# Attention projection by copied token halves, and folds moved to GpSimd

## The reference, cut to what matters

```
def _attn_ref(q, k, v, w_phi):                 # q, k, v: (4, 8, 576, 64), w_phi: (64, 128)
    def phi(x):
        proj = np.einsum('bhsd,df->bhsf', x, w_phi)
        proj = proj - np.max(np.abs(proj), axis=-1, keepdims=True)
        return np.concatenate([np.exp(proj), np.exp(-proj)], axis=-1)
    q_p, k_p = (phi(q), phi(k))
    kv = np.einsum('bhsf,bhsd->bhfd', k_p, v)
    z = np.sum(k_p, axis=2)
    num = np.einsum('bhsf,bhfd->bhsd', q_p, kv)
    den = np.einsum('bhsf,bhf->bhs', q_p, z)[..., None] + 1e-06
    return (num / den).astype(np.float32)
def reference(**kwargs):                       # sequence 576, model width 512
    attention, then x = x + real(fft2(x)) and a channel MLP of width 2048 over its normed rows,
    then a token MLP of width 256, then a channel MLP of width 1536
```

## Time and profile before

| | us |
|---|---|
| median of 3 runs | 994.19 (993.21 to 994.72) |
| the profiled execution's own time | 993.24 |
| its span in the trace | 991.4 |
| PE busy | 976.3 (98%) |
| PE weight loads busy | 879.4 (89%) |
| DVE, ACT, POOL busy | 380.3, 285.3, 181.6 |

### The profile page before, as it was taken

One profiled execution on the slowest core, in us unless ns is written; L12 is line 12 of the kernel. 1 busy time (PEld: TensorE's weight loads), 2 busy tenths in 40 slices (PEclk: granted clock), 3 DMA queues, 4 the chain that ended last, 5 costly groups with the idle time before them and its releaser, 6 DMA issues.

```text
span 991.4 us, 17316 instructions
## 1 busy us (share of the span) xinstructions
PE 976.3 (98%) x7275; PEld 879.4 (89%) x7275; DVE 380.3 (38%) x758; ACT 285.3 (29%) x573; POOL 181.6 (18%) x159
## 2 busy tenths in 40 slices
PE   8999999999999999999999999999999999999998
PEld 6999999888899999899899999788999999999997
DVE  6998888851421322313213213463121212121211
ACT  6865756633311111111111112353111111111110
POOL 3653555369500000000000000136000000000000
PEclk9999999999999999999999999999999999999999
DMA  7232241435310010010100300695010101000000
GB/s 230 80 111 55 74 130 48 165 110 166 108 64 1 1 64 1 1 63 0 37 26 0 105 7 1 208 322 197 1 64 1 64 1 51 13 33 30 32 1 32
DMA packets 48398, 66.88 MB, mean 67 GB/s; under 512 B 22864, under 2 KB 23888, under 8 KB 48208
## 3 DMA queue, kind: packets, MB, share of 16 engines
q1 hardware_dynamic: 46608, 59.69, 18.6%
q10 hardware_dynamic: 1728, 6.29, 1.7%
HBM read 47.10 MB, written 18.87 MB: 67 GB/s over the span
## 4 chain that ended last, share of the span: by engine, by line
PE 73%; POOL 2%; DMA 1%; DVE 1%; ACT 0%; issue 0%; SPq 0%; POOLq 0%
PE mlp_y L1086 11%; PE mlp_y L1087 11%; PE mlp_hid L1073 11%; PE mlp_hid L1071 11%; PE mlp_hid L1072 11%; PE mlp_y L1085 11%; PE mlp_turn_in L1056 1%; PE tok_y L1387 1%; PE tok_y L1389 1%; PE tok_y L1388 1%; POOL mlp_w_lo L1033 1%; DMA mlp_w_raw<-in_w_mlp 1%; PE tok_hid L1389 1%; PE tok_hid L1388 1%; PE tok_hid L1387 1%; DMA tok_w<-in_w_tok 0%
## 5 line engine op out<-in xcount | busy, mean ns | idle before, releaser
L1204 DVE SCALAR_TENSOR_TENSOR mlp_h_lo<-mlp_hid,mlp_h_hi 128x384 fp32r<-128x384 f32 x168 | 93.7, 558 | 465.1 <-ACT mlp_h_hi L1121 465.0
L1071 PE MATMUL mlp_hid<-mlp_ut_hi,mlp_w_hi 128*128 128x384 f32 x672 | 229.1, 341 | 0.5 <-POOL mlp_w_lo L1033 0.5
L1121 ACT ACTIVATE mlp_h_hi<-mlp_hid 128x384 fp32r<-128x384 f32 x168 | 82.7, 492 | 502.9 <-PE mlp_hid L1073 502.9
L1073 PE MATMUL mlp_hid<-mlp_ut_hi,mlp_w_lo 128*128 128x384 f32 x672 | 226.5, 337 | 0.0
L1072 PE MATMUL mlp_hid<-mlp_ut_lo,mlp_w_hi 128*128 128x384 f32 x672 | 225.4, 335 | 0.0
L1085 PE MATMUL mlp_y<-mlp_w_hi,mlp_h_hi 128*128 128x512 f32 x504 | 197.3, 391 | 3.0 <-DVE mlp_h_lo L1204 2.9
L1087 PE MATMUL mlp_y<-mlp_w_hi,mlp_h_lo 128*128 128x512 f32 x504 | 199.4, 396 | 0.0
L1086 PE MATMUL mlp_y<-mlp_w_lo,mlp_h_hi 128*128 128x512 f32 x504 | 198.9, 395 | 0.0
L1033 POOL TENSOR_TENSOR mlp_w_lo<-mlp_w_raw,mlp_w_hi 128x1024 fp32r<-128x1024 f32 x26 | 61.7, 2395 | 402.9 <-ACT mlp_w_hi L1282 381.6
L1071 PEld LDWEIGHTS mlp_hid<-mlp_ut_hi,mlp_w_hi 128*128 128x128 f32 x672 | 126.3, 188 | 6.6 <-issue 1.2
L1072 PEld LDWEIGHTS mlp_hid<-mlp_ut_lo,mlp_w_hi 128*128 128x128 f32 x672 | 126.3, 188 | 5.2
(11 more groups left out here) (146 smaller groups left out, 1081.9 us busy)
## 6 DMA issues: line engine op xcount, KB each, us to landing
mlp_u<-u_scratch SPq DMA_DIRECT2D x12, 768.0 KB, 4.6
mlp_w_raw<-in_w_mlp SPq DMA_DIRECT2D x14, 512.0 KB, 5.2
mlp_w_raw<-in_w_mlp ACTq DMA_DIRECT2D x12, 512.0 KB, 6.0
v<-in_v SPq DMA_DIRECT2D x16, 320.0 KB, 3.6
qk<-in_kT SPq DMA_DIRECT2D x16, 288.0 KB, 4.1
qk<-in_qT SPq DMA_DIRECT2D x15, 288.0 KB, 4.2
u_scratch<-x_all SPq DMA_DIRECT2D x4, 1024.0 KB, 4.9
x_scratch<-mlp_u SPq DMA_DIRECT2D x5, 768.0 KB, 3.6
```

The source lines that it names most:

```text
L1071: nc.tensor.matmul(out, w_hi[:, j, col], hi, start=(c == 0), stop=False)
L1073: last = nc.tensor.matmul(out, w_lo[:, nf - 1 - j, col], hi, start=False, stop=(c == DC - 1))
L1121: nc.scalar.activation(h_hi[:, j % 2, :], hid[j % 2][:, 0:BT], ACT.Relu).then_inc(h_rounded, 1)
L1204: nc.vector.scalar_tensor_tensor(out=h_lo[:, j % 2, :], in0=hid[j % 2][:, 0:BT], scalar=0.0, in1=h_hi[:, j % 2, :], op0=ALU.max, op1=ALU.s ...
```

## The change

The projection of every pair but the first takes another form. SP copies the rounded tokens of each head, from the 64 rows where they lie, to both halves of the 128 rows of new buffers (`rest_twice`, `key_twice`, `query_twice`): four transfers for each of three groups, twelve for a pair. A new weight matrix `wphi_both` has the high part over the low part, 128 rows by 128 columns. A tile is now multiplied in three products: low tokens by `wphi_hi` (256 columns, as before), and for each head its copied tokens by `wphi_both` (128 columns each). PE waits for the copies of REST, of the keys and of the queries. `rest_twice` has two buffers, the others one.

DVE's two folds of `x_all` go to POOL (`pool_fold`), but for the last pair's. POOL's additions of one batch's results move: the second from steps k % 4 = 0 to 1, the third and the row from 1 to 2, the latter two ahead of the fold. SP stores the first batch at pair 13 in place of 11, and the second behind the load of the first MLP's block.

PE's queue in step 0, from the first projection of pair 1 on: before, each tile has three products of 256 columns (L299 is the third).

Two folds came in, and the addition went to the next step. The diff, without the lines that only follow from it:

```
--- before.py
+++ after.py
@@ -116,6 +116,13 @@
+    wphi_both = at("wphi_both", [128, F], F32R, 157824)
+    rest_twice = at("rest_twice", [128, 2, 2, 128], F32R, 134912)
+    key_twice = at("key_twice", [128, 2, 512], F32R, 130816)
+    query_twice = at("query_twice", [128, 2, 512], F32R, 77824)
...
@@ -151,6 +158,9 @@
+    rest_copied = [sem("rest_copied0"), sem("rest_copied1")]
+    key_copied = sem("key_copied")
+    query_copied = sem("query_copied")
...
@@ -236,6 +242,25 @@
         else:
             sp.wait_ge(ones_set, 3)
         sp.dma_start(v[:, p.parity, :, :, 0:DH], dram["v"][p.n]).then_inc(v_loaded[p.parity], 16)
+    def copy_twice(sp, p, first, to, done):
+        for h in range(2):
+            for half in range(2):
+                from_ = qk_hi[DH * h:DH * h + DH, p.parity, first:first + to.shape[2]]
+                sp.dma_start(to[64 * half:64 * half + 64, h, :].bitcast(F32), from_.bitcast(F32)).then_inc(done, 16)
+    def copy_rest(sp, p):
+        wait_if(sp, proj_done, 5 * p.n - 9 if p.n >= 3 else 0)
+        sp.wait_ge(qk_rounded, 2 * p.n + 2)
+        copy_twice(sp, p, FIRST[REST], rest_twice[:, p.parity], rest_copied[p.parity])
+    def copy_keys(sp, p):
+        wait_if(sp, proj_done, 5 * p.n - 2 if p.n >= 2 else 0)
+        copy_twice(sp, p, FIRST[KA], key_twice, key_copied)
+    def copy_queries(sp, p):
+        wait_if(sp, proj_done, 5 * p.n if p.n >= 2 else 0)
+        copy_twice(sp, p, FIRST[QA], query_twice, query_copied)
     def store(sp, b):
         sp.wait_ge(added, FRONT * b + FRONT)
@@ -255,16 +280,24 @@
         load_v(sp, Pair(0))
         load_v(sp, Pair(1))
         load_qk(sp, Pair(2))
+        sp.wait_ge(qk_rounded, 3)
+        copy_keys(sp, Pair(1))
+        copy_rest(sp, Pair(1))
+        copy_queries(sp, Pair(1))
         sp.dma_start(table[:, :], dram["table"]).then_inc(table_loaded, 16)
         for n in range(2, PAIRS):
             if n + 1 < PAIRS:
                 load_qk(sp, Pair(n + 1))
+            copy_rest(sp, Pair(n))
+            copy_keys(sp, Pair(n))
             load_v(sp, Pair(n))
-            if n in (11, 15):
-                store(sp, n // 4 - 2)
+            copy_queries(sp, Pair(n))
+            if n == 13:
+                store(sp, 0)
         sp.wait_ge(qk_split, 2 * PAIRS)
         sp.wait_ge(u_stored[0], 32)
         mlp1["load_block"](sp, 0)
+        store(sp, 1)
         sp.wait_ge(u_stored[1], 32)
         mlp1["load_early"](sp)
         sp.wait_ge(kv_done, PAIRS)
@@ -288,15 +321,29 @@
             pe.wait_ge(qk_split, 1 if unit == REST else 2)
         elif unit == REST:
             pe.wait_ge(qk_split, 2 * p.n + 2)
+        if p.n > 0 and unit == REST:
+            pe.wait_ge(rest_copied[p.parity], 64 * ((p.n + 1) // 2))
+        if p.n > 0 and unit == KA:
+            pe.wait_ge(key_copied, 64 * p.n)
+        if p.n > 0 and unit == QA:
+            pe.wait_ge(query_copied, 64 * p.n)
         wait_if(pe, shifted, 5 * p.n + unit - 1)
         out_bank = proj[(p.parity + unit) % 2]
+        twice = {REST: rest_twice[:, p.parity], KA: key_twice, KB: key_twice, QA: query_twice, QB: query_twice}[unit]
         for j in range(1 if unit == REST else 2):
             tokens = slice(FIRST[unit] + 128 * j, FIRST[unit] + 128 * j + 128)
             hi, lo = qk_hi[:, p.parity, tokens], qk_lo[:, p.parity, tokens]
             out = out_bank[:, 2 * F * j:2 * F * j + 2 * F]
-            nc.tensor.matmul(out, hi, wphi_hi[:, :], start=True, stop=False)
-            nc.tensor.matmul(out, hi, wphi_lo[:, :], start=False, stop=False)
-            last = nc.tensor.matmul(out, lo, wphi_hi[:, :], start=False, stop=True)
+            if p.n == 0:
+                nc.tensor.matmul(out, hi, wphi_hi[:, :], start=True, stop=False)
+                nc.tensor.matmul(out, hi, wphi_lo[:, :], start=False, stop=False)
+                last = nc.tensor.matmul(out, lo, wphi_hi[:, :], start=False, stop=True)
+                continue
+            first = 256 * (unit in (KB, QB)) + 128 * j
+            nc.tensor.matmul(out, lo, wphi_hi[:, :], start=True, stop=False)
+            for h in range(2):
+                last = nc.tensor.matmul(out[:, F * h:F * h + F], twice[:, h, first:first + 128], wphi_both[:, :],
+                                        start=False, stop=(h == 1))
         last.then_inc(proj_done, 1)
     def pe_turn(pe, p, which):
...
@@ -585,6 +634,7 @@
+        nc.scalar.copy(wphi_both[0:DH, :], wphi[0:DH, 0:F]).then_inc(wphi_rounded, 1)
@@ -658,38 +708,20 @@
                 last = nc.vector.tensor_scalar(out, src[rows, 0, 4, 0:DH], rden[rows, 0, 4:5], None, ALU.mult)
         last.then_inc(x_done, 1)
-    def dve_sum(dve, p):
-        b, i = p.n // 4, p.n % 4
-        cols = slice(2 * DH * i, 2 * DH * i + 2 * DH)
-        dve.wait_ge(x_done, p.n + 1)
-        if b > 0:
-            dve.wait_ge(fold_split, 2 * b - 1)
-        x = x_of(b)
-        nc.vector.tensor_tensor(fold_s[:, :, cols], x[:, 0:FRONT, cols], x[:, 5:2:-1, cols],
-                                ALU.add).then_inc(summed, 1)
-    def dve_even(dve, b, i):
-        dve.wait_ge(summed, 4 * b + 3 + i)
-        low, high = MIRROR[i]
-        nc.vector.tensor_tensor(fold_s[:, :, low], fold_s[:, :, low], fold_s[:, :, high],
-                                ALU.add).then_inc(even_folded, 1)
-    def dve_fold(dve, p):
-        dve_sum(dve, p)
-        if p.n % 4 >= 2:
-            dve_even(dve, p.n // 4, p.n % 4 - 2)
     def dve_last_fold(dve):
         cols = slice(D - 2 * DH, D)
         dve.wait_ge(x_done, PAIRS)
+        dve.wait_ge(odd_folded, 2 * B - 1)
         x = x_of(LAST)
         nc.vector.tensor_tensor(fold_d[:, :, cols], x[:, 0:FRONT, cols], x[:, 5:2:-1, cols],
                                 ALU.subtract).then_inc(last_differed, 1)
         nc.vector.tensor_tensor(fold_s[:, :, cols], x[:, 0:FRONT, cols], x[:, 5:2:-1, cols],
                                 ALU.add).then_inc(summed, 1)
-        dve_even(dve, LAST, 1)
         low, high = MIRROR[1]
+        dve.wait_ge(summed, PAIRS)
+        nc.vector.tensor_tensor(fold_s[:, :, low], fold_s[:, :, low], fold_s[:, :, high],
+                                ALU.add).then_inc(even_folded, 1)
         dve.wait_ge(last_differed, 1)
         dve.wait_ge(edge_made, 2 * B)
         nc.vector.tensor_tensor(fold_d[:, :, low], fold_d[:, :, low], fold_d[:, :, high],
@@ -734,16 +766,11 @@
                     dve_low(dve, k // 4 - 1, 0)
                     dve_low(dve, k // 4 - 1, 1)
                 dve_norm(dve, Pair(k - 1))
-                for n in ready(k):
-                    if k < PAIRS - 1:
-                        dve_fold(dve, Pair(n))
             if s == 4 and k == PAIRS - 2:
                 mlp1["early_vector"][0](dve)
             if s == 0 and k == PAIRS - 1:
                 dve.wait_ge(proj_done, 5 * PAIRS)
                 mlp1["early_vector"][1](dve)
-            if s == 4 and k == PAIRS - 1:
-                dve_fold(dve, Pair(k - 1))
     def vector(dve):
         nc.vector.memset(warm[:, :], 0.0).then_inc(warm_set, 1)
@@ -756,6 +783,8 @@
+        nc.vector.tensor_tensor(wphi_both[DH:128, :], wphi[DH:128, F:2 * F], wphi_hi[DH:128, F:2 * F],
+                                ALU.subtract).then_inc(wphi_split, 1)
@@ -789,17 +818,21 @@
     def pool_fold(pool, p):
         b, i = p.n // 4, p.n % 4
         cols = slice(2 * DH * i, 2 * DH * i + 2 * DH)
-        pool.wait_ge(summed, p.n + 1)
-        if i >= 2:
-            pool.wait_ge(even_folded, 2 * b + i - 1)
+        pool.wait_ge(x_done, p.n + 1)
         if b > 0:
             pool.wait_ge(fold_split, 2 * b)
         x = x_of(b)
+        nc.gpsimd.tensor_tensor(fold_s[:, :, cols], x[:, 0:FRONT, cols], x[:, 5:2:-1, cols],
+                                ALU.add).then_inc(summed, 1)
         nc.gpsimd.tensor_tensor(fold_d[:, :, cols], x[:, 0:FRONT, cols], x[:, 5:2:-1, cols],
                                 ALU.subtract).then_inc(differed, 1)
         if i >= 2:
+            low, high = MIRROR[i - 2]
+            pool.wait_ge(summed, p.n + 1)
+            nc.gpsimd.tensor_tensor(fold_s[:, :, low], fold_s[:, :, low], fold_s[:, :, high],
+                                    ALU.add).then_inc(even_folded, 1)
             pool.wait_ge(differed, p.n + 1)
-            low, high = MIRROR[i - 2]
+            pool.wait_ge(even_folded, 2 * b + i - 1)
             o = fold_d[0:1, TILE_OF[0]]
             if i == 3:
                 nc.gpsimd.tensor_copy(edge[:, 0:257:256], o[:, 0:257:256])
@@ -844,15 +877,15 @@
         if k == PAIRS - 1:
             pool.wait_ge(*mlp1["first_normed"])
             mlp1["gpsimd"](pool, (), 0, 2)
+        if k % 4 == 2 and b >= 1:
+            pool_add(pool, b - 1, 2)
+            pool_row(pool, b - 1)
+        if k > 0:
+            pool_fold(pool, Pair(k - 1))
         if k % 4 == 3 and 0 <= b < LAST - 1:
             pool_add(pool, b, 0)
-        if k % 4 == 0 and b >= 1:
+        if k % 4 == 1 and b >= 1:
             pool_add(pool, b - 1, 1)
```

(9 more changed lines are left out.)

## The result

The changed kernel takes 1001.54 us (median of 5 runs, 1000.06 to 1004.07) against 994.19; the ratio is 1.008 with an interval of 1.0068 to 1.0091. The prediction said 991.7, within 986.5 to 999.0. It has the sign wrong, and the time lies outside the range. The trace of the kernel after is of the slowest of its five executions, 1004.07 us, so what is read from it adds up to more (10.8 us of span) than the medians differ (7.4).

The account below looks back on a forecast made before the run. PE was taken to set the pace, with DVE close behind. Projection -2.4, waits on DVE -2.1 and startup +2.0 summed to -2.5 us, so the median 994.19 would become 991.7 us, range 986.5 to 999.0.

Parts of the forecast that it names:

- projection: PE's projection tiles in fifteen pairs: 0.337 us a tile instead of 0.351, plus earlier unit ends; -2.4 us in all.
- waits on DVE: PE's waits behind DVE's folds in steps 4, 5, 9 and 13 go when the folds move; -2.1 us.
- POOL: POOL takes the folds, one or two us more a step, within its room; priced at nothing.
- startup: Pair 1's REST copies land late and PE stalls near 13 us; +2.0 us, lower clock possible but not counted.
- copies in running steps: SP's queue in later steps: twelve copies and three loads fit within 9.55 us and land in time; priced at nothing.
- end of the front: Last pair's folds, pair 14's fold and the first MLP's early weights: nothing, with 1 us either way.
- The narrow product was not slow: Rival in the projection: fp32r products under 256 columns cost 0.244 us, about 1028 us in all; chance 0.13.
- the cheap rival: Rival in the projection: the load is hidden, a narrow product costs 0.058 us, about 978 us in all; chance 0.05.
- The sign for step 9: In the changed kernel's profile step 9 lasts 10.5 to 10.8 us, with no wait on DVE behind REST.
- The slack of 7.9 us: From the keys' release in step 1 to their need in the next step; issues and landing leave 2.6 us or more.
- Startup and copies eat the gain: Rival: clock falls back, REST's copy lands at 16.0, DVE waits become other waits; 996.6 us, chance 0.18.
- The copies are late in every step: Rival: copies land after more than 6.2 us, 2.9 us lost in each of 14 steps, about 1034 us; chance 0.04.

Follow-up runs that it names:

- experiment 2: The changed kernel without any copy, narrow products reading the rounded tokens where they lie (values not the reference's): 988.81 us, ratio 0.9953 to the kernel before.
- experiment 1: The changed kernel with the old projection for every pair and no copies, so only folds, additions and stores moved: 990.99 us, ratio 0.9978.
- experiment 6: The changed kernel with the old projection for pair 1 and no copies for it, twelve copies for each later pair: 996.08 us, ratio 1.0025.
- experiments 3 and 5: 3: changed kernel with six 128-row copies a pair, same bytes, 991.73 us; 5: changed kernel with REST and pair 1 in old form, eight copies, 989.8 us.
- Experiments 7: Old projection with the folds moved, as in experiment 1, but all twelve copies of a pair issued and read by nobody: 997.15 us, ratio 1.0043.
- experiment 8: The changed kernel with REST in its old form for every pair, keys and queries copied from pair 1 on: 995.58 us, ratio 1.0023.
- experiment 10: Experiment 6 with values loaded for the first four pairs only and reused by the others (attention not the reference's): 994.37 us, ratio 1.0013.

## Why the prediction was wrong, by its own steps

| term | predicted | measured | from |
|---|---|---|---|
| projection | -2.4 | -2.2 to -2.5 | experiment 2 against 1 |
| waits on DVE | -2.1 | -2.2 (-1.3 to -3.1); 1.7 of it in steps 4, 5, 9, 13 | experiment 1 |
| POOL | 0 | within the line above | experiment 1 |
| startup | +2.0 | +5.5 | kernel after against experiment 6 |
| copies in running steps | 0 | +7.3 | experiment 6 against 2 |
| end of the front | 0 | not to be told | the traces |
| sum | -2.5 | about +8 | |

Each line is the difference of one run to the next, from the kernel before over experiments 1, 2 and 6 to the kernel after, so that the lines add up says nothing by itself. Behind the last numerators the twelve traces last 792.6 to 794.0 us, in no order that follows the change.

*The projection* was right in its mechanism, and in size for a step without a piece: 0.34 us a tile, 9.30 us a step. Of its parts the tile gained less (0.011 us, 1.5 in all, forecast 1.9) and the earlier end of a group more; and in steps 5, 9 and 13 the gain was eaten by PE's wait for DVE's `x_all`. The narrow product was not slow. Two of them start only 0.06 us apart, as the cheap rival had it, but that buys nothing, since the tile follows its three loads. The load of the stationary tokens, 0.11 us, explains that pace; no run here took the load away.

*The folds* were right in place: waits went in steps 4, 5, 9 and 13, with room on POOL. In size the agreement is partly luck. Each step with one piece gained 0.31 us, not 0.54, and step 4 0.74, not 0.5, which makes 1.7; the rest of the 2.2 lies within the interval. I had put the whole 0.54 of such a step to DVE, although the row for step 9 has PE busy for 11.07 us of 11.29, which leaves 0.22 of standing. The sign for step 9 (10.5 to 10.8 us) failed for this reason and the one above.

*The copies in a running step* are the step that failed, in the sentence "A transfer holds SP's queue for 0.43 us, twelve take 5.2 and three loads about 1.5, within 9.55". The 0.43 came from one row, the table's, a load from HBM. Its neighbour ahead was a load of tokens; behind another copy an entry holds the queue for 0.60, 0.64 with the gap, and sometimes for 1.0 to 1.85 (18 of 180). Twelve are 8.1 us on average, about 10.4 with the loads and gaps, which is more than a plain step. I had let the unknown operation take the price of the nearest known one without bounding it from above; at 0.75 us, a time that the trace of before had for its loads of keys right behind values, the queue would have been full, and this rival would have had a price. The slack of 7.9 us that I worked out from the earlier trace rows was of no use, because a copy isn't issued when its buffer is free but when the queue comes to it. And the low share of DMA (0.36) was the wrong thing to look at: experiments 3 and 5 have 0.77 and 0.85 and lose nothing in running steps.

*Startup* was mis-sized for the same reason and lacked a part. The last of REST's copies went out at 14.0 instead of 12.4, and pair 1's REST started 2.9 us later than before (16.12 against 13.20), not 2.0; PE stood for 3.6. The lower clock followed, which I had named as possible and not counted. What I had not seen is what stands behind the copies: of the queue I had followed the table alone, not the tokens of pair 3, for whose rounding ACT holds back its exponentials. Nor had I seen that the table, sent later, would move just when pair 2's copies and pair 3's tokens need the DMA engines. Experiments 7 and 8 show that this costs 5 to 6 us without any wait for REST: in 7 through pair 3's tokens, in 8 mainly through pair 2's keys, issued in time and landed up to 8.0 us later.

The rival "Startup and copies eat the gain" had the right sign and place, at 996.6 too small. "The copies are late in every step" asked for landings of more than 6.2 us. In step 1 there were such landings, up to 7.3 us; in the later steps that lose, the copies are late mainly by late issue. (Its time is about 1032 by its own terms, 991.7 and 14 times 2.9, not 1034.) Between REST's wait, pair 3's tokens and the lower clock I can't divide the startup's 5.5 us exactly.

## What to carry to other kernels

Before adding transfers to a queue, count its entries in the shortest step, price each by an entry of the trace that has the same neighbour ahead of it (here 0.60 us behind a small copy, 0.43 to 0.47 behind a load of tokens, 0.75 behind values), and compare the sum with the step, since a queue that is full turns every slack into lateness. Name each load that then stands behind the new ones, and follow it to the engine that has it in its queue ahead of other work. If a large transfer moves, look for what lands behind it. Fewer transfers of the same bytes, or leaving the smallest gain out (REST's four copies for one tile), kept the good part here.

## What the runs showed of the hardware

- How long an entry held SP's queue followed the entry ahead of it: behind a copy from SBUF to SBUF 0.60 us (median) for the next copy, at 32, 64, 128 and 256 KB and on 64 or 128 rows alike, and 0.59 for tokens and the table; behind a load of tokens 0.47 for a copy and, in the kernel before, 0.43 for the table. About one entry in ten took over 0.9 us, in the kernel before (5 of 61) as in the one after (23 of 239).
- One fp32r product of 256 columns and two of 128, each with its own stationary operand, took 0.34 us; three of 256 took 0.351. The two narrow ones started 0.06 us apart, and the weight loads 0.11 to 0.12: the loads set the pace, and halving the columns of two products saved 0.011 us.
- Transfers issued right behind one of 1512 KB landed late: four copies of 128 KB took 7.5 to 8.0 us in experiment 8, against a median of 2.8 over the kernel after.
- PE's standing was often followed by a stretch at 1.2 GHz: the startup wait of 3.61 us by 0.57 on average from 16.10 to 20.10 us, one of 1.8 us in step 5 by 0.88 over that step. In experiment 10 one of 2.0 us was followed by none.
- With one load moved to another queue the kernel was 4.8 us slower. The worst wait in its trace, 3.06 us, stood where that load went out just ahead of the keys' copies; that this is the whole cause is not shown.
